# Attention inputs laid out on the host: q and k loaded transposed, v in padded overlapping key blocks

## The chip, the cores and the metric

The kernel runs on one core of one Trainium2 chip. The metric is the device time of one execution in microseconds. The engines are TensorE (PE in the profile; its weight loads are PEld), VectorE (DVE), ScalarE (ACT), GpSimd (POOL) and SyncE (SP), which issues all DMAs.

## What is computed

An attention of two scales, then two feed-forward blocks. All is float32; B, H, S, D = 4, 8, 576, 64, factor 4.

```python
q_d = q.reshape(B, H, S // 4, 4, D).mean(axis=3)      # and k_d, v_d
out_d = sm_attn(q_d, k_d, v_d)                         # 144 x 144 scores per head
out_up = np.repeat(out_d, 4, axis=2)
mask = np.abs(pos[:, None] - pos[None, :]) < 4         # a band of 7 keys
out_local = softmax(where(mask, q k^T / 8, -1e9)) @ v
x = (out_up + out_local)                               # as 2304 tokens x 512
h = x @ w_in1; x = layernorm(h * softmax(h)) * g @ w_out1      # 512 -> 1024 -> 512
h = x @ w_in2; out = (h * cos(h)) @ w_out2                     # 512 -> 2048 -> 512
```

## The kernel before

The program has three stages: attention, the first feed-forward block (`solu_step`), the second (`cos_step`). Each engine has its own instruction stream, written out by hand, and semaphores order them. The change touches the attention alone, which is also the stage in which the weights of the first block are loaded and split.

Attention works on 16 pairs of heads (32 heads, two to a pair: one on partitions 0 to 63, one on 64 to 127). The band is cut into 9 blocks of 64 queries, each against a window of 70 keys (64 and 3 on each side). The engines are software-pipelined by pair; `attention_step` number i does, on TensorE and in this order: `group_scores(i-2)` (L1074), the transposes of the probabilities of pair i-3 (L1083, L1092), the transposes of the k rows of pair i-1 (L1054), the results of pair i-3 in two parts (L1101 with L1116, then L1101 again), the transposes of the q rows of pair i (L1054), and `scores(i-1)` (L1064). "A period" below is one such step. Steps 4 to 15 are a loop; steps 16 to 18 are interleaved with the first steps of the feed-forward block.

The steps that matter, by engine:
- SyncE, `load_rows` (L304): for q and for k two DMAs of 512 rows of 256 bytes (one per head) and one for the last 64 rows, into `rows`; then `vrows` (L315). `load_vwin` (L317): six DMAs of 256-byte rows that build the overlapping windows of v in `vwin`, whose padding is zeroed once by VectorE. 13 DMAs for each pair.
- TensorE, `transpose_rows` (L1048): five transposes for q and five for k, into the first two banks of PSUM. `scores` (L1058) waits for their copies and for the masks two steps back. `group_scores` (L1068) waits for the sums over groups of 4 (`qk_summed`, from GpSimd), for the exponentials of the pair before, and for `out_added`, VectorE's last two instructions for the pair two before. The second part of the results waits for the group exponentials (`gexp_ready`).
- ScalarE, `copy_qT` (L512, two activations L519) and `copy_kT` (L523, L528) take the transposed rows out of PSUM; in its order come the copies of the transposed probabilities (L549, L554), `local_exp` (L532), `group_exp` (L540), `copy_kT`, `copy_group_out` (L562), `split_w1` (L565), `copy_qT`.
- GpSimd sums rows in fours: `sum_v` (L403, L408), `sum_k` (L438, L443), `group_probs` (L449), `sum_q` (L421, L431).
- VectorE: mask, maxima, shift (L789 to L806), then sums and reciprocals (L820 to L834; L823 is the first that needs the group exponentials), `split_w1` (L854), `probs` (L838) and `add_scales` (L848, two instructions), whose end is `out_added`.

Of the kernel before, what the change touches and what calls it, by code (L numbers as in the profile page):

```python
# [10 lines left out]
ds = bass.ds  # L33
# [33 lines left out]
V_LOADS = 6  # L67
# [16 lines left out]
def two_scale_attention_moe(nc, q, k, v, w_in1, w_out1, g_ln, w_in2, w_out2, out):  # L84
    ctx = ExitStack()
    with ctx:
# [51 lines left out]
        rows = [place(f"rows{n}", [P, 2, FULL + 1, 2 * D], F32, at) for n in range(2)]  # L138
# [6 lines left out]
        kT = place("kT", [P, S + 2 * PAD], F32, at)  # L145
# [38 lines left out]
        rowsT_ps = ps[:, 0:2, :].rearrange("p b c -> p (b c)")  # L184
# [20 lines left out]
        rows_loaded = [[sem(f"{w}_rows_loaded{n}") for n in range(2)] for w in "qk"]  # L205
# [7 lines left out]
        rowsT_ready = sem("rowsT_ready")  # L213
        rowsT_copied = sem("rowsT_copied")
# [60 lines left out]
        v_rows = v.rearrange("b h (c p r) d -> p (b h c) (r d)", c=2, r=FACTOR)  # L275
        heads_of_pair = 2 * S * D

        def full_rows(src, head):
            return bass.AP(tensor=src.tensor, offset=head * S * D, ap=[[D, P], [P * D, FULL], [1, D]])

        def tail_rows(src, pair):
            return bass.AP(tensor=src.tensor, offset=pair * heads_of_pair + FULL * P * D,
                           ap=[[D, TAIL], [S * D, 2], [1, D]])

        def v_window(first_key, pair, head, partitions, inner):
            return bass.AP(tensor=v.tensor, offset=pair * heads_of_pair + head * S * D + first_key * D,
                           ap=[[D, partitions]] + inner + [[1, D]])

# [14 lines left out]
        def _(sp):  # L303
            def load_rows(i, n):  # L304
                for w, src in enumerate((q, k)):

                    need(sp, rowsT_ready, 2 * (i - 2) + w + 1)
                    for h in range(2):
                        sp.dma_start(rows[n][:, w, 0:FULL, h * D:(h + 1) * D],
                                     full_rows(src, 2 * i + h)).then_inc(rows_loaded[w][n], DMA)  # L310
                    sp.dma_start(rows[n][0:TAIL, w, FULL, :].rearrange("p (h d) -> p h d", h=2),
                                 tail_rows(src, i)).then_inc(rows_loaded[w][n], DMA)

                need(sp, v_summed, i - 1)
                sp.dma_start(vrows[n][0:GC, :, :], v_rows[:, ds(4 * i, 4), :]).then_inc(vrows_loaded[n], DMA)  # L315

            def load_vwin(i, n):  # L317

                need(sp, out2_ready, i - 1)
                if isinstance(i, int) and i < 2:  # L320

                    sp.wait_ge(pads_set, 7)
                for h in range(2):
                    sp.dma_start(vwin[n][0:WIN, h, 1:NBLK - 1, :],
                                 v_window(BLK - PAD, i, h, WIN, [[BLK * D, NBLK - 2]])).then_inc(vwin_loaded[n], DMA)
                both = [[S * D, 2]]
                sp.dma_start(vwin[n][PAD:PAD + BLK, :, 0, :], v_window(0, i, 0, BLK, both)).then_inc(vwin_loaded[n], DMA)
                sp.dma_start(vwin[n][PAD + BLK:WIN, :, 0, :],
                             v_window(BLK, i, 0, PAD, both)).then_inc(vwin_loaded[n], DMA)
                sp.dma_start(vwin[n][0:BLK, :, NBLK - 1, :],  # L330
                             v_window(S - BLK - PAD, i, 0, BLK, both)).then_inc(vwin_loaded[n], DMA)
                sp.dma_start(vwin[n][BLK:WIN - PAD, :, NBLK - 1, :],
                             v_window(S - PAD, i, 0, PAD, both)).then_inc(vwin_loaded[n], DMA)

            def attention_step(it, n):
                i = 2 * it + n
                load_rows(i, n)
                if exists(i - 1, PAIRS):
                    load_vwin(i - 1, 1 - n)
# [3 lines left out]
            load_rows(2, 0)  # L343
            for c in range(KC):
                sp.dma_start(raw1[:, 2 * c:2 * c + 2, :], w_in1_v[:, c, :, :]).then_inc(raw1_loaded[0], DMA)
            load_vwin(1, 1)
            load_rows(3, 1)
# [3 lines left out]
            load_vwin(2, 0)  # L351
            with sp.Fori(2, PAIRS // 2) as it:
                for n in range(2):
                    attention_step(it, n)
            load_vwin(PAIRS - 1, 1)
# [21 lines left out]
        def _(pool):  # L377
# [33 lines left out]
            def sum_q(i, n):  # L411

                pool.wait_ge(rowsT_copied, 3 * i + 2)
# [11 lines left out]
                need(pool, gscores_ready, i - 1)  # L425
                two = pairs[:].rearrange("p (c g r) -> p c g r", g=GQ, r=2)
# [7 lines left out]
            def sum_k(i):  # L434
                pool.wait_ge(rowsT_copied, 3 * i + 3)
                pool.wait_ge(qk_summed, 3 * i + 2)
                src = kT[:, PAD:PAD + S].rearrange("p (g r) -> p g r", r=2)
                nc.gpsimd.tensor_tensor(pairs[:], src[:, :, 0], src[:, :, 1], ALU.add).then_inc(k_pairs_summed, 1)  # L438
                pool.wait_ge(k_pairs_summed, i + 1)

                need(pool, gscores_ready, i)
                two = pairs[:].rearrange("p (g r) -> p g r", r=2)
                nc.gpsimd.tensor_tensor(kgT[:], two[:, :, 0], two[:, :, 1], ALU.add).then_inc(qk_summed, 1)  # L443
# [7 lines left out]
            def attention_step(it, n):  # L451
                i = 2 * it + n
                if exists(i - 1, PAIRS):
                    sum_v(i - 1, 1 - n, it + n - 1)
                    sum_k(i - 1)
                if exists(i - 2, PAIRS):
                    group_probs(i - 2, n)
                if exists(i, PAIRS):
                    sum_q(i, n)
# [51 lines left out]
        def _(act):  # L511
            def copy_qT(i, n):  # L512
                act.wait_ge(rowsT_ready, 2 * i + 1)

                need(act, scores_ready, i - 1)
                need(act, q_pairs_summed, 2 * (i - 1))
                for h in range(2):
                    half = slice(h * D, (h + 1) * D)
                    nc.scalar.activation(qT[n][half, :, h * BLK:(h + 1) * BLK],  # L519
                                         rowsT_ps[half, 0:S].rearrange("p (j q) -> p j q", q=BLK),  # L520
                                         ACT.Copy).then_inc(rowsT_copied, 1)

            def copy_kT(i):  # L523
                act.wait_ge(rowsT_ready, 2 * i + 2)

                need(act, scores_ready, i)
                need(act, k_pairs_summed, i)
                nc.scalar.activation(kT[:, PAD:PAD + S], rowsT_ps[:, 0:S], ACT.Copy).then_inc(rowsT_copied, 1)  # L528

# [38 lines left out]
            def attention_step(it, n):  # L568
# [3 lines left out]
                if isinstance(i, int) and i == 2:  # L572

                    copy_kT(i - 1)
# [3 lines left out]
                if exists(i - 1, PAIRS) and not (isinstance(i, int) and i == 2):  # L578
                    copy_kT(i - 1)
# [10 lines left out]
                if exists(i, PAIRS):  # L590
                    copy_qT(i, n)
# [4 lines left out]
            act.wait_ge(pads_set, 5)  # L596
# [186 lines left out]
        def _(dve):  # L783
# [96 lines left out]
            nc.vector.memset(qT[0][:], 0.0).then_inc(pads_set, 1)  # L880
            nc.vector.memset(kT[:], 0.0).then_inc(pads_set, 1)
            nc.vector.memset(qgT[0][:], 0.0).then_inc(pads_set, 1)
            nc.vector.memset(qT[1][:], 0.0).then_inc(pads_set, 1)
            nc.vector.memset(qgT[1][:], 0.0).then_inc(pads_set, 1)
            for n in range(2):
                nc.vector.memset(vwin[n][:], 0.0).then_inc(pads_set, 1)
# [160 lines left out]
        def _(pe):  # L1047
            def transpose_rows(i, n, w, turn):  # L1048
                pe.wait_ge(rows_loaded[w][n], 3 * DMA * (turn + 1))

                need(pe, rowsT_copied, 3 * i + 2 * w)
                for c in range(FULL + 1):
                    count = min(P, S - c * P)
                    last = nc.tensor.transpose(rowsT_ps[:, c * P:c * P + count], rows[n][0:count, w, c, :],  # L1054
                                               ident[0:count, 0:count])
                last.then_inc(rowsT_ready, 1)

            def scores(i, n):  # L1058
                pe.wait_ge(rowsT_copied, 3 * i + 3)

                need(pe, masked, 2 * i)
                for j in range(NBLK):
                    at = (j % 5) * WIN
                    last = nc.tensor.matmul(scores_ps[j // 5][:, at:at + WIN], qT[n][:, j, :],  # L1064
                                            kT[:, j * BLK:j * BLK + WIN], start=True, stop=True)
# [41 lines left out]
            def results_first(i, n, turn):  # L1107
                pe.wait_ge(prT_copied, 5 * i + 5)
                pe.wait_ge(vwin_loaded[n], V_LOADS * DMA * (turn + 1))
# [17 lines left out]
            def attention_step(it, n):  # L1127
# [6 lines left out]
                if exists(i - 1, PAIRS):  # L1134
                    transpose_rows(i - 1, 1 - n, 1, it + n - 1)
# [3 lines left out]
                if exists(i, PAIRS):  # L1139
                    transpose_rows(i, n, 0, it)  # L1140
                if exists(i - 1, PAIRS):
                    scores(i - 1, 1 - n)
# [63 lines left out]
            pe.wait_ge(rowsT_copied, 3 * PAIRS)  # L1206
# [97 lines left out]
```

## Time and profile before

| | |
|---|---|
| three runs | 795.8, 796.81, 798.3 us; median 796.81 |
| profiled execution | span 793.5 us from first to last instruction; its own device time isn't listed apart, so the 3.3 us from the span to the median stand for what lies around a span |
| attention up to the last `group_scores` | to 161.4 us of the span |
| first feed-forward block | from 161 us, its last attention steps between |
| PE, PEld busy | 97%, 86% of the span |
| DVE, ACT, POOL busy | 55%, 47%, 22% |
| DMA | 72242 packets, 37.04 MB; 61200 packets under 512 bytes |

The shares of busy time are averages over three stages, and the matmul stages fill most of the span; what the attention stage is limited by is read from its own stretch, from the chain of waits there and from the timeline.
### The profile page before, as it was taken

How to read it: one execution, taken by the hardware profiler on the slowest of the kernel's cores; microseconds unless marked ns; L12 is line 12 of the kernel's file. 1: busy time of each engine (PE TensorE's matmuls, PEld its weight loads, DVE VectorE, ACT ScalarE, POOL GpSimd, SP SyncE). 2: the span in 40 equal slices, each digit the busy share in tenths (PEclk: the TensorE clock that was granted, in tenths of full speed). 3: DMA queues.
4: the chain of work that ended last, by engine and by line, in shares of the span. 5: the costliest groups of instructions: out<-in, count | busy, mean ns of one | idle time of the engine just before them, and what ended most of it. 6: DMA issues, size and time to landing. Idle time of an engine off the chain costs nothing.

```text
span 793.5 us, 13455 instructions
## 1 busy us (share of the span) xinstructions
PE 767.9 (97%) x4656; PEld 682.3 (86%) x4656; DVE 438.7 (55%) x865; ACT 371.0 (47%) x754; POOL 177.7 (22%) x200
## 2 busy tenths in 40 slices
PE   5989999899999999999999999999999999999998
PEld 4777777777999898989999999999999999999997
DVE  4658788847634436273297744544544554464453
ACT  3647777636524334244375544443434444344343
POOL 6658888812201111011001000100100100010010
PEclk9989999989999999999999999999999999999999
DMA  8955665407600000000000010010001001001001
GB/s 168 274 121 127 133 136 132 95 4 199 226 1 1 1 0 0 0 0 1 1 1 1 0 41 1 1 40 0 1 1 40 1 0 40 0 0 40 0 0 40
DMA packets 72242, 37.04 MB, mean 47 GB/s; under 512 B 61200, under 2 KB 65808, under 8 KB 71696
## 3 DMA queue, kind: packets, MB, share of 16 engines
q1 hardware_dynamic: 72208, 36.59, 18.1%
q8 instruction: 21, 0.34, 0.2%
q14 instruction: 13, 0.11, 0.0%
HBM read 31.85 MB, written 4.72 MB: 46 GB/s over the span
## 4 chain that ended last, share of the span: by engine, by line
PE 87%; ACT 4%; issue 3%; DVE 2%; SPq 2%; DMA 1%; DVEq 0%; ACTq 0%
PE ps L1243 25%; PE ps L1258 25%; PE ps L1185 13%; PE ps L1159 12%; PE ps L1064 3%; PE ps L1074 2%; PE ps L1166 2%; ACT gpr L540 2%; PE ps L1092 2%; PE ps L1083 1%; ACT prT L549 1%; PE ps L1054 1%; DMA rows<-in_q 1%; PE ps L1101 1%; DVE xT L848 1%
## 5 line engine op out<-in xcount | busy, mean ns | idle before, releaser
L1009 DVE TENSOR_SCALAR whole<-turn 128x384 f32<-128x384 f32 x96 | 45.9, 478 | 159.7 <-ACT turn L727 159.6
L1243 PE MATMUL ps<-y_hi,wi_lo 128*128 128x384 f32 x384 | 129.5, 337 | 0.0
L1243 PE MATMUL ps<-y_hi,wi_hi 128*128 128x384 f32 x384 | 129.4, 337 | 0.0
L1243 PE MATMUL ps<-y_lo,wi_hi 128*128 128x384 f32 x384 | 129.0, 336 | 0.0
L727 ACT ACTIVATE turn<-ps,quarter 128x384 f32<-128x384 f32 x96 | 55.5, 578 | 144.8 <-PE ps L1243 144.8
L1258 PE MATMUL ps<-wo_hi,g_lo 128*128 128x512 f32 x288 | 113.9, 396 | 0.0
L1258 PE MATMUL ps<-wo_lo,g_hi 128*128 128x512 f32 x288 | 113.7, 395 | 0.0
L1258 PE MATMUL ps<-wo_hi,g_hi 128*128 128x512 f32 x288 | 111.9, 389 | 0.0
L502 POOL TENSOR_TENSOR y_lo<-xT,y_hi 128x1536 fp32r<-128x1536 f32 x7 | 24.5, 3505 | 384.9 <-ACT y_hi L668 384.9
L732 ACT ACTIVATE turn<-turn 128x384 f32<-128x384 f32 x96 | 50.5, 526 | 74.2 <-DVE turn L1012 74.2
L1243 PEld LDWEIGHTS ps<-y_hi,wi_hi 128*128 128x128 f32 x384 | 72.2, 188 | 4.4 <-issue 0.3
L1243 PEld LDWEIGHTS ps<-y_lo,wi_hi 128*128 128x128 f32 x384 | 72.1, 188 | 4.0
L1243 PEld LDWEIGHTS ps<-y_hi,wi_lo 128*128 128x128 f32 x384 | 72.0, 188 | 0.0
L1258 PEld LDWEIGHTS ps<-wo_hi,g_lo 128*128 128x128 f32 x288 | 54.0, 187 | 11.5
L1258 PEld LDWEIGHTS ps<-wo_lo,g_hi 128*128 128x128 f32 x288 | 54.0, 187 | 9.2
L1258 PEld LDWEIGHTS ps<-wo_hi,g_hi 128*128 128x128 f32 x288 | 54.1, 188 | 8.7
L1017 DVE TENSOR_TENSOR turn<-ps,turn 128x384 f32<-128x384 f32 x96 | 53.5, 557 | 12.4 <-ACT turn L732 0.6
L1012 DVE TENSOR_TENSOR turn<-turn,whole 128x384 f32<-128x384 f32 x96 | 53.6, 558 | 3.3
L1185 PE MATMUL ps<-ln_hi,w_hi 128*128 128x384 f32 x160 | 53.6, 335 | 0.0
L1185 PE MATMUL ps<-ln_hi,w_lo 128*128 128x384 f32 x160 | 53.5, 335 | 0.0
L1185 PE MATMUL ps<-ln_lo,w_hi 128*128 128x384 f32 x160 | 53.5, 334 | 0.0
L1022 DVE TENSOR_TENSOR g_lo<-turn,g_hi 128x384 fp32r<-128x384 f32 x96 | 52.9, 551 | 0.6 <-ACT g_hi L738 0.6
(113 smaller groups left out, 1395.2 us busy)
## 6 DMA issues: line engine op xcount, KB each, us to landing
vrows<-in_v SPq DMA_DIRECT2D x16, 288.0 KB
result<-o_sb SPq DMA_DIRECT2D x18, 256.0 KB, 2.1
rows<-in_q SPq DMA_DIRECT2D x32, 128.0 KB, 2.4
rows<-in_k SPq DMA_DIRECT2D x32, 128.0 KB, 2.4
raw_i<-in_moe_w_in SPq DMA_DIRECT2D x4, 1024.0 KB, 10.0
raw_o<-in_moe_w_out SPq DMA_DIRECT2D x4, 1024.0 KB, 11.5
vwin<-in_v SPq DMA_DIRECT2D x32, 122.5 KB
raw<-in_moe_w_in SPq DMA_DIRECT2D x4, 512.0 KB, 5.9
```

The lines of the kernel that those rows point to most:

```text
L502: nc.gpsimd.tensor_tensor(y_lo[n][:], xT[:, :, ds(g * GTOK, GTOK)], y_hi[n][:].bitcast(F32), ALU.subtract).then_inc(y_lo_ready, 1)
L727: nc.scalar.activation(turn[s % 2][:], hT_ps[s % 4], ACT.Identity, bias=quarter[:], scale=INV_2PI).then_inc(turns_ready, 1)
L732: nc.scalar.activation(turn[s % 2][:], turn[s % 2][:], ACT.Sin, scale=TWO_PI).then_inc(cos_ready, 1)
L1009: nc.vector.tensor_scalar(whole[s % 2][:], turn[s % 2][:], ROUND, -ROUND, ALU.add, ALU.add).then_inc(whole_ready, 1)
L1012: nc.vector.tensor_tensor(turn[s % 2][:], turn[s % 2][:], whole[s % 2][:], ALU.subtract).then_inc(frac_ready, 1)
L1017: nc.vector.tensor_tensor(turn[s % 2][:], hT_ps[s % 4], turn[s % 2][:], ALU.mult).then_inc(hcos_ready, 1)
L1022: nc.vector.tensor_tensor(g_lo[s % 4][:], turn[s % 2][:], g_hi[s % 4][:].bitcast(F32), ALU.subtract).then_inc(g_lo_ready, 1)
L1064: last = nc.tensor.matmul(scores_ps[j // 5][:, at:at + WIN], qT[n][:, j, :], kT[:, j * BLK:j * BLK + WIN], start=True, stop=True)
L1159: last = nc.tensor.matmul(h_ps[n][:, f, :], x[n][:, c, :], w[:, 2 * c + f, :], start=(c == 0 and x is x_hi and w is w1_hi), stop=(c == KC ...
L1185: last = nc.tensor.matmul(x2_ps[c % 2], w[:, FC1 + f, c * P:(c + 1) * P], x[:, f, :], start=(f == 0 and w is w1_hi and x is hi), stop=(f = ...
L1243: last = nc.tensor.matmul(hT_ps[s % 4], w[:, j, c, :], x[y][:, c, :], start=(c == 0 and w is wi_hi and x is y_hi), stop=(c == KC - 1 and w ...
L1258: last = nc.tensor.matmul(o_ps[t], x[s % 4][:, t * P:(t + 1) * P], w[:, j, :], start=(j == 0 and x is g_hi and w is wo_hi), stop=(j == FC2 ...
```

## The change

The host hands over q and k already transposed (64 rows of D, per head, by 576 positions), v grouped for the sums, and v cut into 9 windows of 70 keys with zeros at the edges. SyncE's DMAs write q into `qT` and k into `kT`, which gets a second buffer. The transposes of the rows, ScalarE's copies of them and their semaphores go. `vwin` needs no zeroing. The 13 DMAs of a pair become 5. `vrows` is loaded one step later than before, with the windows, and `load_qk` waits for the scores and sums of the pair two before. The loop of SyncE over the steps is written out.

```diff
+QK_LOADS = 3
-        rows = [place(f"rows{n}", [P, 2, FULL + 1, 2 * D], F32, at) for n in range(2)]
-        kT = place("kT", [P, S + 2 * PAD], F32, at)
+        kT = [place(f"kT{n}", [P, S + 2 * PAD], F32, at) for n in range(2)]
...
-            def load_rows(i, n):
-                for w, src in enumerate((q, k)):
-                    need(sp, rowsT_ready, 2 * (i - 2) + w + 1)
-                    for h in range(2):
-                        sp.dma_start(rows[n][:, w, 0:FULL, h * D:(h + 1) * D], ...)
-                    sp.dma_start(rows[n][0:TAIL, w, FULL, :]..., tail_rows(src, i))
+            def load_qk(i, n):
+                need(sp, scores_ready, i - 1)
+                need(sp, q_pairs_summed, 2 * (i - 1))
+                need(sp, k_pairs_summed, i - 1)
+                if isinstance(i, int) and i < 2:
+                    sp.wait_ge(pads_set, 4)
+                for h in range(2):
+                    half = slice(h * D, (h + 1) * D)
+                    sp.dma_start(qT[n][half, :, h * BLK:(h + 1) * BLK],
+                                 q[ds(i, 1), half, :, :].squeeze(0)).then_inc(qk_loaded[n], DMA)
+                sp.dma_start(kT[n][:, PAD:PAD + S], k[ds(i, 1), :, :].squeeze(0)).then_inc(qk_loaded[n], DMA)
+
+            def load_v(i, n):
                 need(sp, v_summed, i - 1)
-                sp.dma_start(vrows[n][0:GC, :, :], v_rows[:, ds(4 * i, 4), :]).then_inc(vrows_loaded[n], DMA)
-            def load_vwin(i, n):
+                sp.dma_start(vrows[n][0:GC, :, :], v_rows[ds(i, 1), :, :, :].squeeze(0)).then_inc(vrows_loaded[n], DMA)
                 need(sp, out2_ready, i - 1)
-                (six DMAs)
+                sp.dma_start(vwin[n][0:WIN, :, :, :], v_windows[ds(i, 1), :, :, :, :].squeeze(0)).then_inc(vwin_loaded[n], DMA)
...
             attention_step(0, 0)
             attention_step(0, 1)
-            load_rows(2, 0)
+            load_v(1, 1)
             for c in range(KC):
                 sp.dma_start(raw1[:, 2 * c:2 * c + 2, :], w_in1_v[:, c, :, :]).then_inc(raw1_loaded[0], DMA)
-            load_vwin(1, 1)
-            load_rows(3, 1)
+            load_qk(2, 0)
+            load_qk(3, 1)
...
-            with sp.Fori(2, PAIRS // 2) as it:
-                for n in range(2):
-                    attention_step(it, n)
+            for i in range(4, PAIRS):
+                attention_step(i // 2, i % 2)
...
-            def sum_q(i, n):
-                pool.wait_ge(rowsT_copied, 3 * i + 2)
+            def sum_q(i, n, turn):
+                pool.wait_ge(qk_loaded[n], QK_LOADS * DMA * (turn + 1))
...
-                pool.wait_ge(rowsT_copied, 3 * i + 3)
                 pool.wait_ge(qk_summed, 3 * i + 2)
...
-            def copy_qT(i, n):
-            def copy_kT(i):
...
-            nc.vector.memset(qT[0][:], 0.0).then_inc(pads_set, 1)
-            nc.vector.memset(kT[:], 0.0).then_inc(pads_set, 1)
-            nc.vector.memset(qgT[0][:], 0.0).then_inc(pads_set, 1)
-            nc.vector.memset(qT[1][:], 0.0).then_inc(pads_set, 1)
-            nc.vector.memset(qgT[1][:], 0.0).then_inc(pads_set, 1)
             for n in range(2):
-                nc.vector.memset(vwin[n][:], 0.0).then_inc(pads_set, 1)
+                nc.vector.memset(qT[n][:], 0.0).then_inc(pads_set, 1)
+                nc.vector.memset(kT[n][:], 0.0).then_inc(pads_set, 1)
+            for n in range(2):
+                nc.vector.memset(qgT[n][:], 0.0).then_inc(pads_set, 1)
...
-            def transpose_rows(i, n, w, turn):
-            def scores(i, n):
-                pe.wait_ge(rowsT_copied, 3 * i + 3)
+            def scores(i, n, turn):
+                pe.wait_ge(qk_loaded[n], QK_LOADS * DMA * (turn + 1))
...
                 if exists(i - 3, PAIRS):
                     transpose_probs(i - 3, 1 - n)
                     transpose_group_probs(i - 3, 1 - n)
-                if exists(i - 1, PAIRS):
-                    transpose_rows(i - 1, 1 - n, 1, it + n - 1)
                 if exists(i - 3, PAIRS):
                     results_first(i - 3, 1 - n, it + n - 2)
                     results_second(i - 3, 1 - n)
-                if exists(i, PAIRS):
-                    transpose_rows(i, n, 0, it)
                 if exists(i - 1, PAIRS):
-                    scores(i - 1, 1 - n)
+                    scores(i - 1, 1 - n, it + n - 1)
...
+def laid_out(q, k, v):
+    windows = np.zeros((PAIRS, 2, S + 2 * PAD, D), v.dtype)
+    windows[:, :, PAD:PAD + S, :] = v.reshape(PAIRS, 2, S, D)
+    windows = np.stack([windows[:, :, j * BLK:j * BLK + WIN, :] for j in range(NBLK)], axis=3)
+    return {
+        "qT": q.transpose(0, 1, 3, 2).reshape(PAIRS, 2 * D, NBLK, BLK),
+        "kT": k.transpose(0, 1, 3, 2).reshape(PAIRS, 2 * D, S),
+        "v_rows": v.reshape(PAIRS, 4, GC, FACTOR * D).transpose(0, 2, 1, 3),
+        "v_windows": windows.transpose(0, 2, 1, 3, 4),
+    }
```

## Rows read from the trace of the kernel before

**Rows 1.** Busy time by stretch: us and instructions of PE, PEld, DVE, ACT, POOL; PEclk; DMA.
```profile
11.00:18.00 7.00, 7.00 (x31) 6.39 (x30) 1.87 (x4) 1.29 (x2) 6.22 (x10) 1.00 0.92 161
19.00:27.00 8.00, 8.00 (x36) 7.28 (x37) 4.96 (x11) 3.36 (x10) 5.99 (x8) 1.00 1.09 312
60.00:150.00 90.00, 84.89 (x924) 67.95 (x924) 73.94 (x150) 65.67 (x171) 76.06 (x90) 1.00 0.61 134
150.00:156.50 6.50, 5.18 (x70) 3.89 (x69) 5.12 (x9) 5.08 (x15) 5.66 (x7) 1.00 0.02 5
156.60:163.40 6.80, 6.80 (x29) 6.32 (x28) 4.80 (x12) 0.73 (x2) 3.53 (x4) 0.50 0.21 47
```
**Rows 2.** Chain of waits, one period of pairs in the loop: start us, us, what.
```profile
103.80 0.94 PE ps L1074 x6
...
112.10 0.80 DVE xT L848 x2
112.94 0.98 PE ps L1074 x6
...
121.97 0.94 PE ps L1074 x6
```
**Rows 3.** Timeline of the same period: start, us, engine, line, what [idle before <-releaser].
```profile
106.23 1.84 POOL L403 TENSOR_TENSOR vpairs<-vrows 72x512 f32<-72x512 f32 x1
...
106.80 0.80 PE L1054 MATMUL ps<-ident,rows 128*128 128x128 f32 x5
...
107.65 0.80 PE L1101 MATMUL ps<-prT,vwin 70*64 70x64 f32 x20
...
108.99 0.64 ACT L528 ACTIVATE kT<-ps 128x576 f32<-128x576 f32 x1
...
109.13 0.70 DVE L823 TENSOR_SCALAR small<-gsum 96x3 f32<-96x3 f32 x1 [0.27 <-ACT gpr L540]
109.15 0.69 PE L1101 MATMUL ps<-prT,vwin 70*64 70x64 f32 x16 [0.21 <-ACT gpr L540]
...
110.56 2.23 PE L1064 MATMUL ps<-kT,qT 128*128 128x70 f32 x18
110.66 1.31 ACT L519 ACTIVATE qT<-ps 64x576 f32<-64x576 f32 x2 [0.24 <-PE ps L1054]
```
**Rows 4.** Timeline, start of the kernel and the first pairs.
```profile
1.09 1.02 DVE L880 MEMSET qT<- 128x1152 f32 x1 [0.22 <-issue]
...
10.04 1.41 PE L1054 MATMUL ps<-ident,rows 128*128 128x128 f32 x5 [1.11 <-DMA rows<-in_q]
...
11.38 4.11 PE L1064 MATMUL ps<-kT,qT 128*128 128x70 f32 x18
...
24.17 1.69 PE L1074 MATMUL ps<-kgT,qgT 128*96 128x144 f32 x6
25.66 1.76 PE L1083 MATMUL ps<-ident,pr 128*70 128x128 f32 x9
...
34.25 0.92 PE L1074 MATMUL ps<-kgT,qgT 128*96 128x144 f32 x6
```
**Rows 5.** Timeline, the pause at 41 us and what follows it.
```profile
43.26 0.87 PE L1054 MATMUL ps<-ident,rows 128*128 128x128 f32 x5 [2.41 <-DMA rows<-in_q]
...
47.97 1.69 PE L1074 MATMUL ps<-kgT,qgT 128*96 128x144 f32 x6
...
54.63 0.69 PE L1101 MATMUL ps<-prT,vwin 70*64 70x64 f32 x16 [0.21 <-ACT gpr L540]
...
58.42 0.98 PE L1074 MATMUL ps<-kgT,qgT 128*96 128x144 f32 x6 [0.16 <-DVE xT L848]
```
**Rows 6.** Timeline, the last period of the attention.
```profile
155.55 0.69 PE L1101 MATMUL ps<-prT,vwin 70*64 70x64 f32 x16 [1.06 <-ACT gpr L540]
...
159.69 1.69 PE L1074 MATMUL ps<-kgT,qgT 128*96 128x144 f32 x6
```
**Rows 7.** DMA issues: name, engine, count, KB each, median us to landing.
```profile
rows<-in_q SPq DMA_DIRECT2D x32, 128.0 KB, 2.4
```

More of the change, by code:

```diff
@@ L66 @@
 DMA = 16
-V_LOADS = 6
+QK_LOADS = 3
 GSCALE = D ** -0.5 / FACTOR ** 2
@@ L81, in need, with two_scale_attention_moe @@
         engine.wait_ge(semaphore, value)
-def two_scale_attention_moe(nc, q, k, v, w_in1, w_out1, g_ln, w_in2, w_out2, out):
+def two_scale_attention_moe(nc, q, k, v_rows, v_windows, w_in1, w_out1, g_ln, w_in2, w_out2, out):
     ctx = ExitStack()
@@ L183, in two_scale_attention_moe @@
         ps = ctx.enter_context(nc.psum_tensor("ps", [P, 8, 512], F32))
-        rowsT_ps = ps[:, 0:2, :].rearrange("p b c -> p (b c)")
         scores_ps = [ps[:, 2, 0:5 * WIN], ps[:, 3, 0:(NBLK - 5) * WIN]]
@@ L204, in two_scale_attention_moe @@
         raw1_loaded = [sem(f"raw1_loaded{n}") for n in range(2)]
-        rows_loaded = [[sem(f"{w}_rows_loaded{n}") for n in range(2)] for w in "qk"]
+        qk_loaded = [sem(f"qk_loaded{n}") for n in range(2)]
         vwin_loaded = [sem(f"vwin_loaded{n}") for n in range(2)]
@@ L212, in two_scale_attention_moe @@
         qk_summed = sem("qk_summed")
-        rowsT_ready = sem("rowsT_ready")
-        rowsT_copied = sem("rowsT_copied")
         scores_ready = sem("scores_ready")
@@ L272, in two_scale_attention_moe @@
         o_stored = [sem(f"o_stored{n}") for n in range(3)]
[L275 to L287, printed above, removed]
         w_in1_v = w_in1.rearrange("(c p) (n m) -> p c n m", p=P, m=512)
@@ L303, in _ @@
         def _(sp):
-            def load_rows(i, n):
-                for w, src in enumerate((q, k)):
-                    need(sp, rowsT_ready, 2 * (i - 2) + w + 1)
-                    for h in range(2):
[L309 to L312, printed above, removed]
+            def load_qk(i, n):
[9 more added lines that the diff above has]
+                sp.dma_start(kT[n][:, PAD:PAD + S], k[ds(i, 1), :, :].squeeze(0)).then_inc(qk_loaded[n], DMA)
@@ L314, in load_rows @@
+            def load_v(i, n):
                 need(sp, v_summed, i - 1)
-                sp.dma_start(vrows[n][0:GC, :, :], v_rows[:, ds(4 * i, 4), :]).then_inc(vrows_loaded[n], DMA)
-            def load_vwin(i, n):
+                sp.dma_start(vrows[n][0:GC, :, :], v_rows[ds(i, 1), :, :, :].squeeze(0)).then_inc(vrows_loaded[n], DMA)
                 need(sp, out2_ready, i - 1)
[L320 to L333, printed above, removed]
@@ L335, in attention_step @@
+                sp.dma_start(vwin[n][0:WIN, :, :, :], v_windows[ds(i, 1), :, :, :, :].squeeze(0)).then_inc(vwin_loaded[n], DMA)
             def attention_step(it, n):
                 i = 2 * it + n
-                load_rows(i, n)
+                load_qk(i, n)
                 if exists(i - 1, PAIRS):
-                    load_vwin(i - 1, 1 - n)
+                    load_v(i - 1, 1 - n)
             attention_step(0, 0)
             attention_step(0, 1)
-            load_rows(2, 0)
+            load_v(1, 1)
@@ L350, in _ @@
                 sp.dma_start(raw1[:, FC1 + c:FC1 + c + 2, :], w_out1_v[:, c:c + 2, :]).then_inc(raw1_loaded[1], DMA)
-            load_vwin(2, 0)
-            with sp.Fori(2, PAIRS // 2) as it:
-                for n in range(2):
-                    attention_step(it, n)
-            load_vwin(PAIRS - 1, 1)
+            load_v(2, 0)
+            for i in range(4, PAIRS):
+                attention_step(i // 2, i % 2)
+            load_v(PAIRS - 1, 1)
             sp.wait_ge(out2_ready, PAIRS)
@@ L425, in sum_q @@
                 need(pool, gscores_ready, i - 1)
+                if isinstance(i, int) and i < 2:
+                    pool.wait_ge(pads_set, 6)
                 two = pairs[:].rearrange("p (c g r) -> p c g r", g=GQ, r=2)
@@ L432, in sum_q, with sum_k @@
                                             two[half, :, :, 1], ALU.add).then_inc(qk_summed, 1)
-            def sum_k(i):
-                pool.wait_ge(rowsT_copied, 3 * i + 3)
+            def sum_k(i, n):
                 pool.wait_ge(qk_summed, 3 * i + 2)
-                src = kT[:, PAD:PAD + S].rearrange("p (g r) -> p g r", r=2)
+                src = kT[n][:, PAD:PAD + S].rearrange("p (g r) -> p g r", r=2)
                 nc.gpsimd.tensor_tensor(pairs[:], src[:, :, 0], src[:, :, 1], ALU.add).then_inc(k_pairs_summed, 1)
@@ L454, in attention_step @@
                     sum_v(i - 1, 1 - n, it + n - 1)
-                    sum_k(i - 1)
+                    sum_k(i - 1, 1 - n)
                 if exists(i - 2, PAIRS):
@@ L458, in attention_step @@
                 if exists(i, PAIRS):
-                    sum_q(i, n)
+                    sum_q(i, n, it)
             for n in range(4):
@@ L511, in _ @@
         def _(act):
-            def copy_qT(i, n):
[L513 to L521, printed above, removed]
-            def copy_kT(i):
[L524 to L528, printed above, removed]
             def local_exp(i, n):
@@ L571, in attention_step @@
                     copy_probsT(i - 3, 1 - n)
-                if isinstance(i, int) and i == 2:
-                    copy_kT(i - 1)
                 if exists(i - 2, PAIRS):
@@ L577, in attention_step @@
                     group_exp(i - 2, n)
-                if exists(i - 1, PAIRS) and not (isinstance(i, int) and i == 2):
-                    copy_kT(i - 1)
                 if exists(i - 3, PAIRS):
@@ L589, in attention_step @@
                     split_w1(i - 3)
-                if exists(i, PAIRS):
-                    copy_qT(i, n)
             act.wait_ge(quarter_set, 1)
             nc.scalar.activation(small[5][:, 0:1], quarter[:], ACT.Exp)
-            act.wait_ge(pads_set, 5)
             for n in range(4):
@@ L1047, in _ @@
         def _(pe):
-            def transpose_rows(i, n, w, turn):
[L1049 to L1056, printed above, removed]
-            def scores(i, n):
-                pe.wait_ge(rowsT_copied, 3 * i + 3)
+            def scores(i, n, turn):
+                pe.wait_ge(qk_loaded[n], QK_LOADS * DMA * (turn + 1))
                 need(pe, masked, 2 * i)
@@ L1063, in scores @@
                     at = (j % 5) * WIN
-                    last = nc.tensor.matmul(scores_ps[j // 5][:, at:at + WIN], qT[n][:, j, :],
-                                            kT[:, j * BLK:j * BLK + WIN], start=True, stop=True)
+                    last = nc.tensor.matmul(scores_ps[j // 5][:, at:at + WIN],
+                                            qT[n][:, j, :], kT[n][:, j * BLK:j * BLK + WIN], start=True, stop=True)
                 last.then_inc(scores_ready, 1)
@@ L1108, in results_first @@
                 pe.wait_ge(prT_copied, 5 * i + 5)
-                pe.wait_ge(vwin_loaded[n], V_LOADS * DMA * (turn + 1))
+                pe.wait_ge(vwin_loaded[n], DMA * (turn + 1))
                 pe.wait_ge(v_summed, i + 1)
@@ L1138, in attention_step @@
                     results_second(i - 3, 1 - n)
-                if exists(i, PAIRS):
-                    transpose_rows(i, n, 0, it)
                 if exists(i - 1, PAIRS):
-                    scores(i - 1, 1 - n)
+                    scores(i - 1, 1 - n, it + n - 1)
             pe.wait_ge(ident_steps, 2)
@@ L1205, in _ @@
             attention_step(PAIRS // 2, 1)
-            pe.wait_ge(rowsT_copied, 3 * PAIRS)
             solu_step(0, 1)
@@ L1283, in _ @@
                 cos_step(GROUPS // 2, s)
-_INS = ["q", "k", "v", "moe_w_in", "moe_w_out", "moe_g_ln", "moe2_w_in", "moe2_w_out"]
+def laid_out(q, k, v):
+    import numpy as np
+    windows = np.zeros((PAIRS, 2, S + 2 * PAD, D), v.dtype)
[7 more added lines that the diff above has]
+    }
+_WEIGHTS = ["moe_w_in", "moe_w_out", "moe_g_ln", "moe2_w_in", "moe2_w_out"]
 def kernel(**inputs):
@@ L1295 @@
     arrays, args = {}, []
-    for name in _INS:
-        a = np.ascontiguousarray(inputs[name])
+    layout = laid_out(inputs["q"], inputs["k"], inputs["v"])
+    for name, a in (*layout.items(), *((name, inputs[name]) for name in _WEIGHTS)):
+        a = np.ascontiguousarray(a)
         arrays[f"in_{name}"] = a
```

## The prediction

> **What bounds the kernel now.** The change touches the attention alone, which ends with the last `group_scores` (L1074) at 161.4 us [rows 6]; so I read that stretch first, by busy time. From 60 to 150 us PE is busy 84.9 of 90 us, and POOL, DVE and ACT 76, 74 and 66 [rows 1]. By this table PE would be the bound, and taking instructions from it would be the way. The chain of waits says something else. In the loop one period of a pair takes (121.97 - 103.80) / 2 = 9.09 us, and the start of L1074 is released every second time by DVE's L848 [rows 2]. The timeline shows the ring: `group_scores`, transposed probabilities, ScalarE's copies and exponentials, which end just before DVE's L823 at 109.13 and PE's L1101 at 109.15; then two branches. PE: second part of the results, q transposes, scores (110.56 + 2.23 = 112.79). DVE: L823 to L848, which ends at 112.90 [rows 2, 3]. The two arrive within 0.1 us of each other. The change shortens the first and not the second.
>
> The other thing to read is PE's clock. PEclk stays at 1.00, that is 2.4 GHz, through the loop [rows 1], but two stretches are at the lower level of 1.2 GHz. The scores of a pair take 4.11 us at the start and 2.23 in the loop, L1074 takes 1.69 and 0.98, five L1054 1.41 and 0.80 [rows 3 to 5]. The start stays at the lower level until about 27 us, although PE's records fill all of 11 to 18 us and all of 19 to 27 us [rows 1].
>
> **The steady period, if the clock stays.** Removed from PE: ten L1054, 0.80 and about 0.79 us. From ACT: the k copy 0.64 and two q copies, 1.31 [rows 3]. None is worth its duration.
> - The k transposes stand before L1101 at 107.65, which also waits for ACT's copy of the group probabilities, ended 107.41: gain 0.13 to 0.2 us for the first part of the results, nothing for the second, which waits for the exponentials at 109.15 [rows 3].
> - The k copy at 108.99 starts after those exponentials; behind it only the group output and the weight split, which DVE needs later. Nothing.
> - The q transposes between L1101 and L1064 are on PE's branch: it gets 0.79 us shorter and ends near 112.0.
> - DVE's branch, 109.13 to 112.90, loses nothing but what POOL's earlier sums leave it. DVE's L823, 3 columns wide, takes 0.70 us because POOL is at work beside it [rows 3]. The Trainium skill (SBUF — State Buffer, "SBUF: two separate sides") calls the shared port an exclusive lock; the row agrees.
>
> So with the clock up, a period is shorter by 0 to 0.25 us; I take 0.13, as POOL follows the results by that much: 8.96 us. PE then stands idle 0.6 to 0.8 us before every L1074. The loads: 13 issues become 5; the q loads remain 256-byte pieces, k and v become long rows. `load_qk(i)` waits for the scores of pair i-2, a whole period before its first user; with three issues of about 0.5 us and 2.4 us to land [rows 7] it lands some 5 us ahead. `vrows` moves behind it and behind that wait: issued 2 us after the scores end, landed some 4.3 us after; POOL's L403 wants it 2.5 us after L1074 starts at 103.76 [rows 2, 3]. It starts up to 1 us late, runs without the overlap that stretches it to 1.84, and is done before L408's own wait for the results. Cost 0, at worst 0.5 us a period if the landing takes 1 us longer; SP queues nothing urgent behind it.
>
> **The clock.** It fell at 156.6 us, in the first step that has no q transposes (no pair is left to load): PE had done the k transposes, the results (L1101) in two parts with 1.06 us of idle between them, and gone straight to the scores; it was busy 5.18 of 6.5 us from 150 [rows 1, 6]. It also fell after the pause of 2.41 us at 41 to 43 us [rows 5]. In the twelve periods of the loop it never fell: there each stretch of small matmuls (L1101 writes 64 columns from 70 rows) has a set of full 128 x 128 transposes before and behind it, and PE waits 0.21 us. The change takes both sets out of exactly this stretch. What is left from the end of L1092 to the scores is 0.5 us idle (waiting for ACT), the small matmuls, 0.3 us idle, more small matmuls; and 0.6 us idle before L1074. That is nearer to 150 to 156 us than to the loop. I expect the clock to fall in the first or second period.
>
> Would it come back? At 11 to 18 and 19 to 27 us a PE without a gap stayed low through transposes and scores; it rose near 27 us, after L1074 and nine L1083 back to back behind scores, and in the second stretch again while L1074 and L1083 ran behind each other [rows 1, 4, 5]. With the change that happens for part of a period only, and the small matmuls follow at once. So it rises seldom and falls again. By the Trainium skill (TensorE: Matmul & The Clock Gate, "What's actually happening") activity releases the throttle; taken as busy time, it would lift the clock where rows 1 show it low, so the rule alone would keep this kernel in the fast case below. The same page ("A second HAM failure mode: psum-queue depth-cycling") has pauses between groups making the clock oscillate, which speaks for this forecast.
>
> **Price of a period at the lower level.** L1074 started 47.97, the second L1101 54.63: 6.66 us, though its last part was at the upper level [rows 5]. Lower bound: 6.66 + 0.6 (L1101 unslowed) + 4.04 (scores to the start of L1074) = 11.3. Upper bound: the first part of the results, 1.3 us, and L1101 grow like the scores, by 1.84: 1.1 and 0.5 more, L1092 0.1 to 0.3 more: 13.0. I take the middle, 12.2; DVE's branch (3.8 after the exponentials) then ends 1.5 us before PE's.
>
> **The start.** Before, the scores of pair 0 start at 11.38 behind rows, transposes and copies [rows 4]. After, SP waits for four memsets (two of 1.02, two about half, from 1.09 [rows 4]): 4.5 us, three issues, 2.4 to land: 8.2. Scores to 12.2; POOL's sums (9 instructions, about 5.8 us from 8.2) let L1074 start at 14.0; scores of pair 1 to 19.7; L1074 and L1083 to 23.4; results, as 24.17 to 30.78 before but lower clock, to 28.8; scores to 32.8. L1074 of pair 2 starts at 32.8 against 34.25 [rows 4]: -1.4 us.
>
> **The sum.** From L1074 of pair 2 (34.25) to that of pair 15 (159.69) are 13 periods: 125.4 us before [rows 4, 6]. After: 13 x 12.2 = 158.6, +33.2. Two or three short spells at the upper level, each worth some 1.6 us: -4. The feed-forward matmuls start at the lower level in both, +0.5. Sum -1.4 + 33.2 - 4 + 0.5 = +28.3. Against the profiled span: 793.5 + 28.3 = 821.8; with the 3.3 us by which the median stands above that span, 825 us. The bounds of the period, 11.3 and 13.0, give 813 and 835; with more or fewer spells 811 to 837 for this case.
>
> **Rivals.**
> - Faster: the clock stays up in the loop. Pair 2 is reached at 30.3 (-3.9), as the clock rises near 27 us; then the stall for q rows, 2.41 us, and the low stretch behind it go, so that the L1074 of pair 4 comes at 48.2 instead of 58.42 (-10.2) [rows 5]; eleven periods at -0.13 make -11.6. Time 785 (782 to 789). For it: the records call PE busy in most of each period even after the change. Against: 11 to 27 us.
> - Mixed: the clock falls in about a quarter to a half of the periods. -11.6 + 13 x 3.2 x 0.25 is about 0; at a half +9: 790 to 811.
> - Between them decides one point: whether the clock falls in the step between the results and the scores. That the removed work isn't removed can't be: the diff drops the instructions.
> - `vrows` late by 1 us more: 13 x 0.5 = +6 on the faster rival, 791; small, within the mixed case.
>
> **Chances.** Lower clock through most of the attention 0.72, clock stays 0.20, mixed 0.08. The likeliest case's own range is 811 to 837. It holds about 0.64, so the range has to reach to the faster rival: 784 to 837. Faster by over 0.3% (about what a measurement of this kernel can tell from no change) 0.23: the rival and a third of the mixed case; within 0.3% 0.02; slower 0.75.
>
> **What would show it.** L1054, L519 and L528 gone. In the loop PEclk 0.50 in most stretches, L1064 near 4.0 us a pair, the period near 12 us, chain of waits through PE alone, first scores near 8 us, no wait for the q rows at 43 us. I'm wrong if PEclk is 1.00 from 60 to 130 us: then L1074 is released by L848 each time and the period is near 9.0. If L403 is seen waiting for a DMA and DVE's branch moves with it, the `vrows` step was wrong.

## The result and the profile after

The changed kernel takes 825.22 us (median of 4 runs, 823.57 to 827.46) against 796.9 before: a ratio of 1.036, 95% interval 1.033 to 1.038. It is slower, by 28.3 us, and the forecast was 825. The profiled execution has a span of 825.5 us and a time of 827.46, the slowest of the four. Its span is 32.0 us longer than the 793.5 us of the kernel before, and these 32.0 us are what the rest of this text divides up.

Section 1 of the page, busy time by engine, shows fewer instructions on the two engines that lost work: PE has 4496 matmuls for 4656, ACT 706 instructions for 754; DVE and POOL have what they had but for one. The page counts 31953 DMA packets for 72242. The DMA issues are fewer and larger, and they land later than the 2.4 us of [rows 7].

```profile
PE 776.9 (94%) x4496; PEld 695.9 (84%) x4496; DVE 437.4 (53%) x864; ACT 342.7 (42%) x706; POOL 171.0 (21%) x200
```
```profile
qT<-in_qT SPq DMA_DIRECT2D x32, 144.0 KB, 3.1
kT<-in_kT SPq DMA_DIRECT2D x16, 288.0 KB, 3.9
```

PE's busy time went up, from 767.9 to 776.9 us, with fewer instructions. The table by stretch says why (columns as in [rows 1]):

```profile
11.00:18.00 7.00, 2.64 (x13) 2.44 (x12) 0.88 (x2) 0.00 (x0) 3.43 (x5) 1.00 0.97 224
...
60.00:130.00 70.00, 61.44 (x507) 52.43 (x505) 46.00 (x93) 29.70 (x86) 41.92 (x54) 0.68 0.40 109
```

The granted clock is 0.68 in the loop, a mixture of 1.2 and 2.4 GHz, where it was 1.00 [rows 1]. That was the forecast, though it had the lower level in most of the loop, with two or three short spells above. Two things were not forecast. From 11 to 18 us PE does 2.6 us of work where it did 7. And the chain of waits (start, us, what) runs every second period through a load; the main pieces of one such passage are

```profile
143.38 4.06 PE ps L975 x18
147.46 0.54 SPq L273
...
149.39 3.73 DMA vrows<-in_v_rows
...
154.68 1.26 POOL vsums L356
155.94 1.20 POOL pairs L387
...
157.77 0.97 PE ps L985 x6
```

The scores end (L975), SyncE issues q, k and then the v rows, these land 5.7 us after the scores' end, POOL sums v and then k, and only then the group scores (L985) start. In the list of waits (us in total, times, longest) POOL's first v sum is held up by its DMA 14 times; the list of the kernel before has no such wait. PE's group scores wait for POOL's k sums (L392) 17.4 us in all:

```profile
POOL vpairs L351 <- DMA vrows<-in_v_rows: 56.4, 14, 9.2
```

The worst of them is at the start: the v rows of pair 2 are issued behind the second 2 MB of weights, and the timeline shows

```profile
41.32 1.26 POOL L351 TENSOR_TENSOR vpairs<-vrows 72x512 f32<-72x512 f32 x1 [9.17 <-DMA vrows<-in_v_rows]
...
44.64 1.75 PE L985 MATMUL ps<-kgT,qgT 128*96 128x144 f32 x6 [7.49 <-POOL kgT L392]
```

The group scores of pair 2 start 10.4 us later than before (34.25 [rows 4]), those of pair 15 30.9 us later (190.55 against 159.69 [rows 6]). So 10.4 us come from the start, 20.5 from the 13 periods behind it (11.22 us each for a mean of 9.65, which takes in the slow periods at 43 and 156 us), 1.1 from the rest of the span.

### The profile page after: what moved, and what is told of

It reads as the page before. It is cut to its first block, busy times and chain, and to the rows that moved or that the text cites. A ratio compares the mean times of both kernels' runs of the same rounds, so it can differ in the third digit from the quotient of the medians.

```text
span 825.5 us, 12546 instructions
## 1 busy us (share of the span) xinstructions
PE 776.9 (94%) x4496; PEld 695.9 (84%) x4496; DVE 437.4 (53%) x864; ACT 342.7 (42%) x706; POOL 171.0 (21%) x200
## 2 busy tenths in 40 slices
DMA packets 31953, 37.07 MB, mean 45 GB/s; under 512 B 21200, under 2 KB 21200, under 8 KB 31408
## 4 chain that ended last, share of the span: by engine, by line
PE 85%; issue 3%; ACT 3%; DMA 2%; POOL 2%; SPq 1%; DVE 1%; POOLq 0%; ACTq 0%; DVEq 0%
PE ps L1149 24%; PE ps L1164 24%; PE ps L1092 12%; PE ps L1066 12%; PE ps L975 4%; DMA vrows<-in_v_rows 2%; PE ps L1073 2%; PE ps L994 2%; PE ps L985 2%; PE ps L1012 2%; PE ps L1003 1%; ACT gpr L471 1%; POOL pairs L387 1%; SPq L273 1%; POOL vsums L356 1%
## 5 line engine op out<-in xcount | busy, mean ns | idle before, releaser
L650 ACT ACTIVATE turn<-ps,quarter 128x384 f32<-128x384 f32 x96 | 55.7, 581 | 144.4 <-PE ps L1149 144.4
L975 PE MATMUL ps<-kT,qT 128*128 128x70 f32 x288 | 58.8, 391 | 9.6 <-DMA kT<-in_kT 9.6
L480 ACT ACTIVATE prT<-ps 70x256 f32<-70x256 f32 (+2 forms) x48 | 22.9, 486 | 102.7 <-PE ps L994 102.1
L975 PEld LDWEIGHTS ps<-kT,qT 128*128 128x128 f32 x288 | 56.1, 299 | 10.8 <-issue 9.5
```

Of the source, the lines that this page charges most:

```text
L480: nc.scalar.activation(prT[0:WIN, first:first + count, :], prT_ps[(n + x) % 2][0:WIN, 0:count * P].rearrange("p (m q) -> p m q", q=P), ACT ...
L650: nc.scalar.activation(turn[s % 2][:], hT_ps[s % 4], ACT.Identity, bias=quarter[:], scale=INV_2PI).then_inc(turns_ready, 1)
```

## The experiments

With a changed clock and a late load in one kernel, the load could be the cause of both: PE stands still behind it, and in the kernel before the clock also fell after a pause of 2.41 us [rows 5]. Theory C is the forecast's (the missing work on PE is enough), theory V this rival (the late v rows are the cause). The first three kernels are the two edits that tell them apart, alone and together.

**e1_v_early.** The v rows go back to a step earlier.

```diff
             def load_qk(i, n):
                 ...
                 sp.dma_start(kT[n][:, PAD:PAD + S], ...)
+                need(sp, v_summed, i - 1)
+                sp.dma_start(vrows[n][0:GC, :, :], ...)
             def load_v(i, n):
-                need(sp, v_summed, i - 1)
-                sp.dma_start(vrows[n][0:GC, :, :], ...)
```

> The changed kernel with one DMA moved: the grouped v rows of pair i are issued right behind q and k of pair i, as in the kernel before, a step earlier than in the change. Theory C (the clock falls because PE lost the row transposes, whatever the loads do): the waits of POOL's first v sum for its DMA (56.4 us in 14 waits) go, the pause at the start goes (-10 us), but PEclk stays at 0.50 for most of the loop and a period is 10.8 to 11.3 us against 9.09 before: 805 to 813 us. Theory V (the clock falls only because PE stands idle behind the late v rows): PEclk is 1.00 from 50 to 150 us, a period is about 9.0 us, 783 to 788 us.

**e2_filler.** Ten idle transposes for each pair, where the row transposes stood: PE transposes the identity, and nobody reads the result.

```diff
+            def filler(count):
+                for c in range(count):
+                    nc.tensor.transpose(ps[:, c // 4, c % 4 * P:(c % 4 + 1) * P], ident[:], ident[:])
...
                     transpose_group_probs(i - 3, 1 - n)
+                if exists(i - 1, PAIRS):
+                    filler(5)
                 if exists(i - 3, PAIRS):
                     results_first(i - 3, 1 - n, it + n - 2)
                     results_second(i - 3, 1 - n)
+                if exists(i, PAIRS):
+                    filler(5)
```

> The changed kernel with ten transposes of the identity for each pair on PE, at the places of the removed row transposes, into the two free PSUM banks; nobody waits for them. v rows late as in the change. Theory C: they hold the clock at 1.00 in most of the loop although they are more work; what is left is the pause at the start (+10 us) and the ring through the late v rows, 10.4 us from the end of the scores to the second next group scores plus 9.0 back, 9.7 us a period: 805 to 812 us. Theory V: the idle behind the late rows is still there, the clock falls as before and PE has 1.6 us more to do in each period: 825 to 845 us.

**e3_both.** Both edits.

> Both edits. Theory C: the clock stays at 1.00 after the start, a period is 9.0 to 9.1 us as before, and the start and the pause at 43 us are shorter by about 10 us: 784 to 789 us, so faster than both kernels. Theory V: 784 to 789 us as well, but then e1_v_early is there too, and this one is up to 2 us slower than it.

Measured, with the starts of the group scores of pair 2 and pair 15 and the mean granted clock from 50 to 150 us of each profiled execution:

| kernel | pair 2 | pair 15 | a period | clock | median us | ratio to before, 95% |
|---|---|---|---|---|---|---|
| before | 34.25 | 159.69 | 9.65 | 1.00 | 796.9 | |
| changed | 44.64 | 190.55 | 11.22 | 0.69 | 825.2 | 1.033 to 1.038 |
| e1_v_early | 37.35 | 179.70 | 10.95 | 0.72 | 815.0 | 1.017 to 1.026 |
| e2_filler | 44.74 | 178.19 | 10.27 | 0.91 | 814.1 | 1.020 to 1.026 |
| e3_both | 37.01 | 161.45 | 9.57 | 0.97 | 793.4 | 0.994 to 0.999 |

Theory V falls: with the v rows early the clock is low for nearly as long as in the change (a mean of 0.72 for 0.69). The idle transposes are 0.71 and 0.77 us more of PE's time a pair (e3_both), some 24 us in all, and take 11.1 us off the changed kernel, 21.6 us off e1_v_early. The late v rows cost 10.2 us on the kernel without the idle transposes and 20.7 us on the one with them: I read this as a part of the wait lying beside PE's slower work in the first case; no run tested that by itself. The times of e1 and e2 lie 2 us above their ranges, e3_both 4 us above its range: in it the clock fell in two pauses of PE, of 3.66 us before 37.01 and 3.90 us before 60.02, while q and k came behind the weights. From 68 to 150 us it was 1.00. The table by stretch of the two kernels that differ in the idle transposes alone, e1_v_early and then e3_both:

```profile
50.00:150.00 100.00, 88.77 (x762) 75.44 (x760) 69.45 (x139) 44.11 (x129) 67.92 (x86) 0.72 0.45 118
```
```profile
50.00:150.00 100.00, 88.19 (x996) 72.99 (x995) 76.21 (x157) 51.65 (x153) 81.60 (x98) 0.97 0.52 133
```

PE is busy for the same 88 us in both and gets 762 matmuls done in one, 996 in the other, 110 of these the idle transposes. PE's timeline of one period of e1_v_early shows where the clock goes:

```profile
122.85 1.69 PE L984 MATMUL ps<-kgT,qgT 128*96 128x144 f32 x6
124.33 2.13 PE L993 MATMUL ps<-ident,pr 128*70 128x128 f32 x9
...
128.16 0.80 PE L1011 MATMUL ps<-prT,vwin 70*64 70x64 f32 x20 [0.68 <-ACT gprT L484]
...
129.67 0.69 PE L1011 MATMUL ps<-prT,vwin 70*64 70x64 f32 x16 [0.21 <-ACT gpr L470]
130.28 4.09 PE L974 MATMUL ps<-kT,qT 128*128 128x70 f32 x18
```

The group scores (L984) are slow, 1.69 us for 0.98 [rows 2], and the transposes at their beginning; behind them the clock is up: L1011, the small matmuls of the results, takes 0.80 and 0.69 us as in [rows 3]; after the small matmuls and two waits the scores are slow again.

**e8_before_bare** is the test without the change: the kernel before, with four of its five row transposes left out in the loop, for q and for k. Most of q and k is then stale, all loads, copies and waits stay.

```diff
-                for c in range(FULL + 1):
+                for c in range(FULL + 1) if isinstance(i, int) else range(1):
```

> The kernel before with four of the five row transposes left out for q and for k in the loop steps (4 to 15); the loads, copies and waits all stay, most of q and k is then stale data of an earlier pair. Theory C: without any change of a load the clock falls to the lower level in many periods, and the kernel becomes slower by doing less: 802 to 815 us. Rival (the clock fell because of the change's loads or waits): PEclk stays 1.00 in the loop and the time is 794 to 797 us.

It took 806.0 us, ratio 1.009 to 1.016. PE does less, nothing else is touched, and the kernel is 9 us slower; the clock from 50 to 150 us is 0.84. PE by stretches of 2 us (busy, PEclk, DMA share, GB/s), with four of the lines of its timeline:

```profile
124.00:126.00 2.00, 1.79 (x42) 0.94 0.67 153
126.00:128.00 2.00, 2.00 (x17) 0.50 0.59 168
128.00:130.00 2.00, 2.00 (x11) 0.50 0.75 130
130.00:132.00 2.00, 2.00 (x11) 0.50 0.32 72
```
```profile
120.04 0.98 PE L1074 MATMUL ps<-kgT,qgT 128*96 128x144 f32 x6 [0.85 <-DVE xT L848]
...
125.44 0.90 PE L1101 MATMUL ps<-prT,vwin 70*64 70x64 f32 x16 [0.21 <-ACT gpr L540]
...
126.54 3.95 PE L1064 MATMUL ps<-kT,qT 128*128 128x70 f32 x18
130.28 1.69 PE L1074 MATMUL ps<-kgT,qgT 128*96 128x144 f32 x6
```

It falls within the second part of the small matmuls (L1101 takes 0.90 us for 0.69), just ahead of the scores. The pauses of PE in that period are 0.85 us before the group scores and 0.57 and 0.21 us before the two parts of the results.

**e4_k_place and e5_q_place.** e3_both with only one of the two sets of idle transposes.

> e3_both with the five idle transposes at the place of the k transposes (before the first part of the results) kept and those at the place of the q transposes left out. Theory C says that PE's work at this place joins the two waits around the small matmuls: the clock stays at 1.00 in most of the loop, period 9.0 us, 791 to 797 us. If both sets are needed (rival), the clock falls in every second or third period: 800 to 812 us.

> e3_both with the five at the place of the q transposes (between results and scores) kept and those at the place of the k transposes left out. Theory C: PE's stretch of small matmuls and two waits before them is bare, as in e1_v_early, so the clock falls often: 803 to 815 us. Rival, that the amount of work alone counts wherever it stands: the same time as e4_k_place within 2 us.

e4_k_place: 798.1 us (0.998 to 1.003), clock 0.91, a period 9.83 us. e5_q_place: 810.3 us (the median of three runs, 807.5 to 816.8; a fourth took 823.2; ratio 1.012 to 1.018), clock 0.71, a period 11.29 us; inside its range. Against e1_v_early, which has none (815.0), the same five transposes are worth 17 us or at most 5, by their place: before the small matmuls, in PE's wait for ACT, they keep the clock up for 82% of the time from 50 to 150 us; behind them they hardly do. e4_k_place lies between its two theories: 1 us above its range, and the clock dips in each of the four periods from 85 to 126 us. Both sets together are 4.7 us better in the medians, but the two intervals overlap.

**e6_order, e7_split_wait, e9_spread** follow the other part of the loss, the start. Each builds on the one before, from e3_both. In e7_split_wait ScalarE's loop is also cut in three, so that step 11 stands by itself (left out here).

```diff
e6_order
             load_v(1, 1)
+            load_qk(2, 0)
             for c in range(KC):
                 sp.dma_start(raw1[:, 2 * c:2 * c + 2, :], ...)
-            load_qk(2, 0)
             load_qk(3, 1)
+            load_v(2, 0)
             sp.dma_start(gs[:, FC1:2 * FC1], ...)
             for c in range(0, FC1, 2):
                 sp.dma_start(raw1[:, FC1 + c:FC1 + c + 2, :], ...)
-            load_v(2, 0)
e7_split_wait
...
-                    else:
+                    if isinstance(i, int) and i == FC1 + 3:
                         act.wait_ge(g_loaded, DMA)
                         act.wait_ge(raw1_loaded[1], FC1 // 2 * DMA)
e9_spread
-            for c in range(0, FC1, 2):
-                sp.dma_start(raw1[:, FC1 + c:FC1 + c + 2, :], ...)
             for i in range(4, PAIRS):
                 attention_step(i // 2, i % 2)
+                c = 2 * (i - 5)
+                if 0 <= c < FC1:
+                    sp.dma_start(raw1[:, FC1 + c:FC1 + c + 2, :], ...)
```

> e3_both with two changes of order in SyncE's start: q, k and v rows of pair 2 before the 2 MB of the first weights instead of behind them, and the windows of pair 2 before the 2 MB of the second weights. In e3_both the scores of pair 2 waited for k until 31.1 us and group scores of pair 2 came at 37.0 us. Theory (the start is limited by loads queued behind the weights): group scores of pair 2 at 28 to 31 us, 784 to 789 us. Rival (the weights are needed as early, so the wait moves to ScalarE's split): no gain, 792 to 796 us.

> e6_order with one wait moved: ScalarE's weight split waits for the second 2 MB of weights from step 11 on, where it first reads them, and not from step 4 on. In e6_order it stood 9.66 us in step 4 for them, and the group scores of pair 4 came at 60.8 us instead of some 52. Theory: with that wait gone group scores of pair 4 at 51 to 53 us, clock at 1.00 from 25 us to the end of the loop, period 9.0 us: 784 to 789 us, faster than the kernel before and the changed one. Rival: the load of pair 4 queued behind the weights takes its place (q and k land late), gain 0 to 3 us: 792 to 796 us.

> e7_split_wait with the four DMAs of the second weights (512 KB each) issued one a step in steps 5 to 8 instead of all in step 3; they are first read in step 11. In e7_split_wait k of pair 4 landed at 49.5 us behind them, PE stood idle 4.3 us and the clock fell at 55.6 us. Theory (a queue in front of q and k): group scores of pair 4 at 50 to 52 us instead of 56.0, clock at 1.00 until the loop's end, 5 us less in the profiled execution: 786 to 790 us. Rival: each 512 KB delays the v rows of its own step by as much, 793 to 796 us.

e6_order: 795.5 us (0.996 to 1.000). Its theory fell, its rival held: pair 2 came at 33.5 us for 37.0 (28 to 31 expected), and then ScalarE's split stood 9.66 us for the second weights. e7_split_wait: 794.7 us (0.995 to 1.000), again the rival: the split no longer waits, but k of pair 4 lands behind those weights. e9_spread, which takes the weights out of the way: 786.9 us (0.984 to 0.989), inside its range and the fastest of all. Its profiled execution, at 792.2 us the slowest of its six, doesn't show how: the clock is 1.00 from 50 to 150 us, but q and k of pair 3 are now the late ones, PE stands 3.32 us before 45.26, and pair 4 comes at 55.7 us, not at 50 to 52, and no earlier than in e7_split_wait (56.0). So the 7.8 us between the medians stand, and their way is open. Nor was the same order of loads tried in the kernel before.

**e10_spread_bare** is e9_spread without the idle transposes.

> e9_spread without the idle transposes: every load early or out of the way, PE as bare as in the change. Theory C: with no wait for a load left that could explain it, the clock still falls in most periods: 805 to 815 us, 18 us or more above e9_spread, which does 16 us more work on PE. Rival (the clock in e1_v_early fell because of pauses for loads at the start, from which it didn't recover): within 3 us of e9_spread.

809.6 us (1.012 to 1.019), clock 0.77: 22.8 us slower than e9_spread, though PE has some 24 us less to do (16 in what was expected). From 60 to 150 us PE stands nowhere longer than 0.82 us, and never for a load; the bare PE loses its clock all the same.

## Why the prediction was right, and which of its steps were not

- **What bounds the loop.** Right. Where the clock holds, e3_both has the period that the two branches give: from 88.54 to 142.67 us six periods of 9.02, against 9.09 before and 8.96 forecast, and the group scores wait for DVE's last instruction. PE's branch is as long there as before, by the idle transposes; no run has the upper level throughout with the shorter branch, so the 0.13 us that I gave it is untested:

```profile
97.60 0.98 PE L988 MATMUL ps<-kgT,qgT 128*96 128x144 f32 x6 [0.32 <-DVE xT L770]
```

  ScalarE's copies, 1.95 us a period [rows 3], were worth next to nothing, as said: it has 51.65 us to do in 100 where it had 72, and the period is 0.07 us shorter.
- **The clock falls.** Right in kind, in place (in the second part of the results or right behind it) and in cause, as e8 and e10 show. The rule of the Trainium skill (TensorE: Matmul & The Clock Gate, "What's actually happening"), that activity releases the throttle, doesn't hold here if activity is read as the busy time of the records: PE is busy 88 of 100 us in e1_v_early at 0.72. Its section "A second HAM failure mode: psum-queue depth-cycling", where short pauses between groups of matmuls make the clock go up and down, fits what was seen: PE pauses 0.68 and 0.21 us a period in e1_v_early.
- **How long it stays down.** Too pessimistic. I took 12.2 us a period with two or three short spells at the upper level. The clock came back in most periods, around group scores and transposes: 0.68 from 60 to 130 us is 36% of the time at the upper level ((0.68 - 0.50) / 0.50). A period without late v rows (e1_v_early) was 10.95 us, below my lower bound of 11.3. The term 13 x 12.2 - 125.4 - 4 = +29.2 measured 13 x 10.95 - 125.4 = +17.0.
- **The v rows cost nothing.** Wrong, and the sign named for it is there: POOL's first v sum (L403 before, L351 now) waits for a DMA 14 times, and the chain runs through it. I let them land 4.3 us after the scores, with the landing time of a 128 KB load [rows 7]; they landed 5.7 us after, as the issues took 2.0 us and the 288 KB 3.7 us. I also asked what the wait costs only for the upper level, where PE would stand idle before the group scores; at the lower level they follow the scores at once, and POOL's k sums, which they need, come behind its v sums. It cost 3.5 us in the loop (13 x 0.27) beside the low clock; with the idle transposes in, e2_filler against e3_both, 0.70 us a period.
- **The start.** Wrong in sign. -1.4 was forecast, +10.4 measured: 3.1 us (e1_v_early, 37.35 us) because q and k of pair 2 come behind the first 2 MB of weights, so that POOL's sums keep PE waiting 1.89 us, and because the scores before them take 4.12 us for 2.23; 7.3 us because its v rows come behind the second (44.64). I counted the issues and not what was queued in front of them. The first steps were late too: scores at 9.56 us for 8.2, group scores of pair 0 at 18.49 for 14.0, behind v rows that landed near 15.2.
- **The sum.** -1.4 + 29.2 + 0.5 = 28.3 forecast; 10.4 + 17.0 + 3.5 + 1.1 = 32.0 measured in the profiled executions, 28.3 in the medians. The mechanism and the sign hold. That the number does is luck: the low clock was put 12.2 us too high, the start and the v rows 15.3 us too low. Of the 3.7 us between the two sums 2.2 are that the slowest execution of the changed kernel was profiled. And the 3.3 us that I added for what lies around a span are about 2.2 in the other executions of the kernel before, so the one with the 793.5 us was some 1 us below its median.

## What to carry to other kernels

Before taking instructions off TensorE, look at what will stand between its waits: if short matmuls with pauses are all that is left, the clock may go, and cost more than the work did. Work for nobody can be put there (ten 128-column transposes a period here, worth 22 and 23 us in two pairs of kernels, 11 us with the v rows late), and its place counts: five of them were worth 17 us in one place and at most 5 in another. With the clock held and the loads spread out, the new layout took 786.9 us against 796.7. A load that moves behind a wait for the scores, or behind 2 MB of weights in the same queue, has to be costed by what is in front of it.

## What the runs showed of the hardware that was not expected

- PE's busy records didn't tell its clock: in e8_before_bare it was busy 2.00 of 2 us in each stretch from 126 to 132 us, at 0.50.
- No long pause was needed: in e8_before_bare the clock fell in about every second period, and the longest pause of PE in the one shown is 0.85 us.
- Larger loads took longer to land: 2.4 us for 128 KB [rows 7], 3.1 for 144, 3.9 for 288 (their pieces and what was queued beside them differ too). What fewer than half the packets (31953 for 72242) are worth by themselves no run shows; e3_both, which has them, is within 1% of the kernel before.
- Why the clock returned in some periods of a kernel and not in others was not tried.
